# A chunked delta rule: full-array products with block masks against small row-tiled products, and inverses from two 16x16 blocks turned by VectorE

## The reference, cut to what matters

```
def _attn_ref(q, k, v, beta):          # 4 batches, 8 heads, 768 tokens, head dimension 48
    k_n = k / (np.linalg.norm(k, axis=-1, keepdims=True) + 1e-06)
    for t in range(S):
        y[:, :, t] = np.einsum('bhd,bhde->bhe', q[:, :, t], state)
        v_old = np.einsum('bhde,bhd->bhe', state, kt)
        state = state + bt[:, :, :, None] * np.einsum('bhd,bhe->bhde', kt, vt - v_old)
...
    x = attn_out as (3072 tokens, 384)
    x = _moe_ref(x, ...)               # x @ w_in, a rational function, @ w_out (384 -> 2048 -> 384)
    return _moe2_ref(x, ...)           # x @ w_in, h * tanh(softplus(h)), @ w_out
```

## Time and profile before

| what | value |
|---|---|
| runs shown | median 1323.81 us, 1314.73 to 1342.42, 3 runs |
| profiled execution | 1310.02 us, of which the span of the trace is 1308.0 us |
| start, to the first residual | 74 us |
| recurrence of 48 steps | 350.3 us |
| feed-forward | 883.7 us |
| busy in the span | TensorE 1151.2 us (88%), VectorE 933.4 (71%), ScalarE 739.5 (57%), GpSimd 194.9 (15%) |
| mean granted clock of TensorE | 0.925 |

### The profile page before, as it was taken

The page is one execution under the profiler, slowest core; times in us unless marked ns, Lnnn a source line. Parts: engine busy times, 40 slices in busy tenths (PEclk is TensorE's granted clock), DMA queues, the critical chain, the costliest instruction groups (busy, mean ns, idle before and its releaser), DMA issues.

```text
span 1308.0 us, 23511 instructions
## 1 busy us (share of the span) xinstructions
PE 1151.2 (88%) x9559; PEld 891.0 (68%) x9612; DVE 933.4 (71%) x1042; ACT 739.5 (57%) x932; POOL 194.9 (15%) x365
## 2 busy tenths in 40 slices
PE   5169697979899889998999999888999899989997
PEld 3146465657666667777777777667878787878875
DVE  2733343433444699998999999998878687768785
ACT  1124242413443777767777777776666566656664
POOL 1518646473820000000000000000000000000000
PEclk6569696958999999999999999999999899999999
DMA  6975565544462110001010102123010101010000
GB/s 141 208 154 121 128 133 143 126 112 111 105 199 64 37 49 18 31 1 48 0 48 0 49 1 82 40 73 97 1 49 1 49 0 48 1 48 1 23 2 25
DMA packets 81694, 83.82 MB, mean 64 GB/s; under 512 B 55040, under 2 KB 62720, under 8 KB 81024
## 3 DMA queue, kind: packets, MB, share of 16 engines
q1 hardware_dynamic: 70880, 60.43, 18.3%
q10 hardware_dynamic: 10720, 22.03, 6.1%
HBM read 61.99 MB, written 20.45 MB: 63 GB/s over the span
## 4 chain that ended last, share of the span: by engine, by line
DVE 31%; PE 29%; ACT 3%; issue 3%; DVEq 0%; ACTq 0%
PE o_ps L825 6%; PE o_ps L827 5%; PE o_ps L826 5%; DVE g_lo L1035 5%; DVE val L1029 5%; DVE val L997 4%; DVE val L1016 4%; PE h_ps L825 4%; PE h_ps L827 4%; PE h_ps L826 4%; DVE den L989 4%; DVE den L1024 4%; DVE pa L995 4%; ACT g_hi L895 1%; ACT stage L931 1%
## 5 line engine op out<-in xcount | busy, mean ns | idle before, releaser
L895 ACT ACTIVATE g_hi<-val 128x1024 fp32r<-128x1024 f32 x96 | 101.9, 1061 | 104.7 <-DVE val L1029 99.1
L825 PE MATMUL o_ps<-g_hi,w_hi_early 128*128 128x512 f32 x288 | 119.0, 413 | 32.2 <-DVE g_lo L1035 31.8
L825 PE MATMUL o_ps<-g_hi,w_hi_late 128*128 128x512 f32 x288 | 117.3, 407 | 22.5 <-DVE g_lo L1035 22.4
L681 DVE TENSOR_TENSOR u_blk<-hz_ps,w_blk 128x768 f32<-128x768 f32 x48 | 46.0, 958 | 116.7 <-PE hz_ps L390 116.7
L1029 DVE SCALAR_TENSOR_TENSOR val<-den,val 128x1024 f32<-128x1024 f32 x96 | 117.7, 1226 | 10.7 <-DVE den L1024 0.5
L525 ACT ACTIVATE stage<-y_ps 128x256 f32<-128x256 f32 x48 | 18.2, 379 | 183.9 <-PE y_ps L422 183.5
L1035 DVE SCALAR_TENSOR_TENSOR g_lo<-val,g_hi 128x1024 fp32r<-128x1024 f32 x96 | 117.6, 1225 | 5.8 <-ACT g_hi L895 5.7
L826 PE MATMUL o_ps<-g_lo,w_hi_early 128*128 128x512 f32 x288 | 116.1, 403 | 0.0
L827 PE MATMUL o_ps<-g_hi,w_lo_early 128*128 128x512 f32 x288 | 115.8, 402 | 0.0
L825 PE MATMUL h_ps<-x_hi,w_hi_early 128*128 128x512 f32 x288 | 112.4, 390 | 2.4 <-DVE val L997 2.0
L826 PE MATMUL o_ps<-g_lo,w_hi_late 128*128 128x512 f32 x288 | 114.3, 397 | 0.0
(11 more groups left out here) (96 smaller groups left out, 2368.5 us busy)
## 6 DMA issues: line engine op xcount, KB each, us to landing
w_raw<-w SPq DMA_DIRECT2D x14, 768.0 KB, 4.4
kq_gram<-kq_t SPq DMA_DIRECT2D x12, 768.0 KB, 11.4
x_raw<-x_dram SPq DMA_DIRECT2D x12, 768.0 KB, 5.5
kq_run<-kq_t ACTq DMA_DIRECT2D x40, 192.0 KB, 3.8
kv_run<-kv_n ACTq DMA_DIRECT2D x20, 384.0 KB, 5.3
k_norm<-kv_n SPq DMA_DIRECT2D x6, 768.0 KB, 4.7
x_dram<-stage ACTq DMA_DIRECT2D x24, 192.0 KB, 4.5
x_dram<-stage SPq DMA_DIRECT2D x6, 768.0 KB, 4.1
```

The source lines that it names most:

```text
L825: nc.tensor.matmul(dst, hi, rhs_hi, start=first, stop=False)
L895: act_fn(g_hi[:, n % 2], val[:, n % 2], ACT.Copy, scale=-1.0).then_inc(g_hi_ready, 1)
```

## The change

- The masks of blocks are gone (x_blk, u_blk, p_blk, w_blk, blk_mask and the work that made them). `solve`, `update` and `within` are instead written as 16 small products a step, one for each head and batch, whose operands lie at the 32 partitions of the batch (`quad(b)`). `update` and `within` are each cut into two halves of 8 products (batches 0 and 1, then 2 and 3), with the batches of a half in different PSUM banks.
- The 32x32 inverse is made from its two 16x16 diagonal blocks (`substitute`, 15 rounds, both blocks at once) and an off-diagonal block that TensorE makes in two products for each matrix (`side_join`, 64 products a call, four calls a tile) with a masked copy by ScalarE (`masked`) between and an addition by VectorE (`join`) behind.
- n_mat is turned into one matrix a partition, and the inverses back, by three VectorE transposes a tile (`turn_n`, `turn_z`, `turn_x`). n_dram and inv_dram are gone.
- The keys and queries are loaded once, in a ring of three tiles (kq), by SyncE, 4 chunks a tile. All loads and stores of the part are in SyncE's queue.
- No `keep_warm` is left in the recurrence. In the start there are 12 + 16 + 16.
- The loops over tiles are written out.
- y is stored to x1 in another order of batches, so a tile of x1 is loaded in pieces of 32 tokens (`load_x1`, 6 DMAs of 1024 pieces of 128 B), and a tile of x2 in 6 DMAs.

```diff
+    def load_x1(self, q, x1, t):
+        for k in range(KT):
+            tokens = self.x_raw[:, k].rearrange("p (m o t) -> p m o t", o=2, t=C)
+            stored = x1[P * k:P * k + P, t].rearrange("p (o m t) -> p m o t", o=2, t=C)
+            for o in range(2):
+                q.dma_start(tokens[:, :, o], stored[:, :, o]).then_inc(self.x_loaded, 16)
...
-            def hand_inverses(tau, first=False, following=True):
...
-                sp.wait_ge(inv_ready, tau + 3)
-                sp.dma_start(inv_dram, inv_x[:].rearrange("p i k -> p (i k)")).then_inc(inv_stored, 16)
...
-                        sp.dma_start(x_blk[C * b:C * b + C, c, :, C * b:C * b + C],
-                                     src[c, b]).then_inc(x_blk_loaded[c], 16)
...
+            for c in range(CT):
+                load_kq(0, c)
+            load_norm(1)
+            for c in range(CT):
+                load_kq(1, c)
+            for c in range(CT):
+                load_kv(0, c)
+            load_norm(2)
+            for c in range(CT):
+                load_kq(2, c)
+            for i in range(2):
+                w.load(sp, w1, i)
+            for tau in range(T):
+                if tau + 3 < T:
+                    load_norm(tau + 3)
...
                 for c in range(CT):
...
+                    if tau + 1 < T:
+                        sp.wait_ge(st_done, index(tau, c, 1) + 1)
+                        load_kv(tau + 1, c)
+                    if tau + RING < T:
+                        load_kq(tau + RING, c)
+                    if c == 1 and tau:
+                        store_y(tau - 1, 1)
+                    if c == 3:
+                        store_y(tau, 0)
+                if tau == 2:
+                    for cp in range(2):
+                        sp.wait_ge(hand.y_stored[cp], 64 + 64)
+                    hand.load_x1(sp, x1, 0)
...
+        def substitute(eng, tt, step, done):
...
+            for r in range(HC - 1, 0, -1):
+                shape = [P, 2, r, HC - r]
+                eng.wait_ge(step, done)
+                tt(inv_t[:, :, 0:r, r:HC], n[:, :, r, 0:r].unsqueeze(3).broadcast_to(shape),
+                   x[:, :, r, r:HC].unsqueeze(2).broadcast_to(shape), ALU.mult).then_inc(step, 1)
+                eng.wait_ge(step, done + 1)
+                tt(x[:, :, 0:r, r:HC], x[:, :, 0:r, r:HC], inv_t[:, :, 0:r, r:HC], ALU.subtract).then_inc(step, 1)
+                done += 2
...
+                pool.wait_ge(x_ready, j)
+                pool.wait_ge(eye_step, 5)
+                nc.gpsimd.tensor_copy(blocks(inv), eye[:]).then_inc(pool_step, 1)
+                pool.wait_ge(n_turned_ready, j + 1)
+                substitute(pool, nc.gpsimd.tensor_tensor, pool_step, STEPS * (j - 1) + 1)
...
+            def side_join(j, k):
...
+                for n in range(CG // 2):
+                    m = CG // 2 * h + n
+                    for b in range(B):
+                        left, right = ((n_mat[quad(b), j % 2, m], z_diag[quad(b), m]) if k % 2 == 0 else
+                                       (r_mat[quad(b), m], x_mat[quad(b), j % 2, m, HC:C]))
+                        last = nc.tensor.matmul(bg_ps[quad(b), 0, HC * n:HC * n + HC], left, right,
+                                                start=True, stop=True)
+                last.then_inc(bg_done, 1)
...
             def solve(tau, c, g):
...
-                for u in range(U):
-                    last = nc.tensor.matmul(hz_ps[:, u], x_blk[:, c, U * g + u], z[:, g, u],
...
+                for r in range(HALVES):
+                    for v in range(V):
+                        for b in range(B):
+                            last = nc.tensor.matmul(kh_ps[quad(b), r, P + D * v:P + D * v + D],
+                                                    x_mat[quad(b), tau % 2, HEADS * c + U * g + V * r + v],
+                                                    z[quad(b), V * r + v], start=True, stop=True)
                 last.then_inc(hz_done, 1)
...
             def q_state(tau, c, g):
...
+                for h in range(2):
+                    for v in range(V):
+                        for o in range(2):
+                            for r in range(HALVES):
+                                last = nc.tensor.matmul(y_at(r, v, 2 * h + o), state[rows(r), g, o, h, v],
+                                                        kq[rows(r), CT * (tau % RING) + c, 1, B * (V * g + v) + 2 * h + o],
+                                                        start=(h == 0 and v == 0), stop=False, skip_group_check=True)
...
+            def update(tau, c, g, h):
+                q = index(tau, c, g)
+                if h == 0:
+                    pe.wait_ge(u_ready, q + 1)
+                    pe.wait_ge(state_ready, q + 2)
+                else:
+                    pe.wait_ge(st_half, q + 1)
+                by_event()
+                for v in range(V):
                     for r in range(HALVES):
...
+                        for b in (2 * h, 2 * h + 1):
+                            at = V * D * h + D * v
+                            last = nc.tensor.matmul(st_ps[rows(r), b % 2, at:at + D], kv[quad(b), c, 0, U * g + V * r + v],
+                                                    u_row[quad(b), V * r + v], start=True, stop=True)
+                last.then_inc(st_done if h else st_half, 1)
+            def within(tau, c, g, h):
+                q = index(tau, c, g)
+                if h == 0:
+                    pe.wait_ge(q_done, q + 1)
...
+                    pe.wait_ge(y_half, q + 1)
+                by_event()
+                for v in range(V):
+                    for r in range(HALVES):
+                        for b in (2 * h, 2 * h + 1):
+                            last = nc.tensor.matmul(y_at(r, v, b), u_row[quad(b), V * r + v],
+                                                    p_mat[quad(b), tau % RING, HEADS * c + U * g + V * r + v],
+                                                    start=False, stop=True, skip_group_check=True)
+                last.then_inc(y_done if h else y_half, 1)
...
-                            gram_fill(tau + 2, G2 * c + g - FIRST_FILL)
-                        keep_warm(4)
-                        solve(tau, c, g)
-                        keep_warm(2)
-                        q_state(tau, c, g)
-                        keep_warm(1)
-                        update(tau, c, g)
-                        before = (c, g)
-                within(tau, *before)
...
+            keep_warm(12, bg_ps)
+            for c in range(CT):
+                early_gram(0, c)
+            pe.wait_ge(early_used, 1)
+            by_event()
+            keep_warm(16, bg_ps)
+            for c in range(3):
+                early_gram(1, c)
+            keep_warm(16, bg_ps)
+            for k in range(4):
+                side_join(0, k)
+                if k == 0:
+                    early_gram(1, 3)
...
+            pe.wait_ge(cleared, 4)
+            k_state(0, 0, 0)
+            for tau in range(T):
+                for s in range(NQ):
+                    c, g = s // G2, s % G2
+                    if s < CT and tau + 2 < T:
+                        side_gram(tau + 2, s)
+                    if s >= CT and tau + 1 < T:
+                        side_join(tau + 1, s - CT)
+                    solve(tau, c, g)
+                    q_state(tau, c, g)
+                    update(tau, c, g, 0)
+                    within(tau, c, g, 0)
+                    if s + 1 < NQ:
+                        k_state(tau, (s + 1) // G2, (s + 1) % G2)
+                    elif tau + 1 < T:
+                        k_state(tau + 1, 0, 0)
+                    within(tau, c, g, 1)
+                    update(tau, c, g, 1)
...
-            def spread_p(c, p):
-                for b in range(B):
-                    last = nc.scalar.activation(p_blk[:, c % 2, :, b], p[:, HEADS * c:HEADS * c + HEADS], ACT.Copy,
-                                                scale=blk_mask[:, b:b + 1])
...
+            def masked(j, h):
...
+                nc.scalar.activation(r_mat[:, CG // 2 * h:CG // 2 * h + CG // 2, 0:HC],
+                                     bg_ps[:, 0, 0:CG // 2 * HC].rearrange("p (n k) -> p n k", k=HC),
+                                     ACT.Copy, scale=lower_rows[:, 0:1]).then_inc(bg_used, 1)
...
+            def scale_gram(j, c, ps):
...
+                    dve_tt(part(n_mat[:, j % 2]), fill[:, 0], ws.unsqueeze(3).broadcast_to(shape), ALU.mult)
+                    last = dve_tt(part(p_mat[:, j % RING]), fill[:, 1],
+                                  upper[:].unsqueeze(1).unsqueeze(1).broadcast_to(shape), ALU.mult)
...
+            def turn_n(j):
...
+                nc.vector.transpose(square(n_turned), n_mat[:, j % 2].rearrange("p n k -> p k n")).then_inc(n_turned_ready, 1)
+            def turn_z(j):
...
+                nc.vector.transpose(z_diag[:].rearrange("p n i -> p i n"), square(inv)[:, 0:HC]).then_inc(z_diag_ready, 1)
+            def turn_x(j):
...
```

(70 more changed lines are left out.)

666 lines of the change are left out of this document (274 added, 392 removed).

## The result

The changed kernel takes 1317.22 us (median of 20 runs, 1311.31 to 1320.04), the kernel before beside it 1327.15 (median of 20, 1301.81 to 1349.25). The ratio of this kernel to the one before is 1.007 with a 95% interval of 1.004 to 1.010; it stands above 1, though the median is lower, because it leaves out runs in a slower state with a lower clock, which the kernel before fell into often. That is 0.7% slower and under the 2% that count as a change, where I had forecast 100 us less. The profiled execution took 1317.5 us, its span 1315.6.

What follows compares the result with a forecast made beforehand. TensorE was taken to bound the recurrence, forecast at 249 + 5 + 10 + 10 = 274 us instead of 350; with the start, 1310 - 76 - 26 = 1208 us, as a median 1222, range 1125 to 1290.

Steps and rivals of the forecast that it cites:

- The stops: Recurrence, TensorE waiting on "issue" in the written-out program of some 6,100 products: 10 us, bounds 0 and 53.
- the stops multiply: Rival, recurrence: stops of 4.4 us twice a tile, 53 us instead of 10, total 1265 us; chance 0.12.
- Products: Recurrence: TensorE's small products at half clock, gram products and off-diagonal groups included, take 249 us.
- products don't overlap in one bank: Rival, recurrence: products at different array rows writing one PSUM bank run one after another, 219 us more, 1441 us; chance 0.08.
- Clock: TensorE in the recurrence: stays at half clock, 1.2 GHz (0.50), giving 1222 us; chance 0.52.
- full-clock rival: Rival, recurrence: the dense stream keeps TensorE at 2.4 GHz, recurrence 185 us, total 1133 us; chance 0.22.
- VectorE and hand-overs: Recurrence: VectorE's work mostly hidden, 5 us showing; hand-overs and drains 0.2 us a step, 10 us.
- Not on the path: Rival, recurrence: another wait keeps the step as long as before, only the start's 26 us come, 1298 us; chance 0.06.
- Start: Before the recurrence: first residual at 48 us, 26 less than before, bounds 42 and 58.
- Feed-forward: Last stage: x1's loads in small pieces stay hidden and cost nothing; uncovered, up to 10 us in each of five tiles.
- The sum: Whole kernel: recurrence 76 us less and start 26 less give 1208 us profiled, 1222 us as a median.

Runs made afterwards that it cites:

- after: The changed kernel itself, against the kernel before it: median 1317.22 us, ratio 1.007.
- all_loop: Changed kernel's products reading fixed buffers, TensorE's recurrence looped over chunks of two steps, not the delta rule: 1204.99 us; the same written out 1309.77 us.
- wide7: Changed kernel with seven wide bf16 products of 512 columns added ahead of every step's side work: 1339.02 us, ratio 1.022.
- probe_stream: Changed kernel with five streams of small products, written out or looped, ahead of everything on TensorE; 1024 fp32 products took 78 us written out, 28.7 us looped.

## Why the prediction was wrong, point by point

- **The stops: the step that failed.** "The written-out program has some 6,100 products against a looped one ... I take 10 us, bounds 0 and 53." The changed recurrence lasts 369.6 us, the same products from a loop 260.2: the stops cost 109 us, twice the upper bound (107 us between the looped kernel and its own control). I had priced them as four rare events of the earlier trace rows and asked how often they would recur, in the rival *the stops multiply* as well (two a tile; "TensorE's program is read at some 130 products a step"). They are not events but a rate: 88 blocks of 256 instructions at 4.2 us each on average (3.5 to 4.0 in the probes), beside 1.9 us for running 64 small products. The rival came nearest to the mechanism, with half its size, since it kept the stop's 4.4 us and guessed the count. The count of blocks was in the diff (5632 x 4 / 256); the time that a block takes was in no row of before.
- **Products.** 249 us of them were forecast; the looped version holds them and every hand-over in 260. `solve` 0.81 (0.76), `q_state` 0.79 (0.89), `k_state` 0.50 (0.50), `update` 0.36 + 0.48 (1.04), gram 1.12 (1.0), off-diagonal groups 1.73 in the looped version (2.0): right within some tenths of a us, and *products don't overlap in one bank* (`solve` 3.0) falls. The Trainium skill (TensorEngine Tiling (Array Packing), "Restrictions and Gotchas", Gotcha 1) says that different row tiles can't access one PSUM bank at the same time. `solve` in 0.81 us disagrees with it, with four row places writing one bank; each of the four writes its own 32 partitions there, and products that share both bank and partitions weren't run.
- **Clock.** 0.50 as forecast, in after and in all_loop, where TensorE is busy 236.5 of 262.3 us. The full-clock rival didn't come, and wide7 with its 0.71 was no faster.
- **VectorE and hand-overs**, 5 + 10 us: 9.5 us of waits for VectorE in all_loop. The transposes were 1.9 to 2.0 us for 1024 elements and not 1.1, hidden as argued.
- **Not on the path.** This rival's 1298 us came nearest by number. That is luck: its mechanism, another wait of the chain between the engines, did not come. VectorE made TensorE wait 2.8 us.
- **Start.** First residual 59.21 us, forecast 48 (bounds 42 and 58). Part of it may be the same step: in the start's gram products TensorE stood 3.8 us at 18.6 and 6.3 us at 34.3 on "issue", while the loads ran (198 GB/s on average over the start). How much of that reached the first residual isn't shown, and the rest, three transposes at 0.9 us more each among it, I haven't split.
- **Feed-forward.** 885.1 us, with 883.7 forecast: the loads of x1 are hidden.
- **The sum.** 1208 for the profiled run, 1317.5 measured: +96 the recurrence, +11 the start, +3 the rest. As a median 1222 was forecast and 1317.2 measured.

Not tried: a looped recurrence that computes the reference. It would need each chunk's K and Q, keys, inverses and masked products brought to fixed buffers, and what those copies cost isn't known from these runs; 1205 us therefore shows what the supply costs, and isn't the time of a kernel that could be used.

## What to carry to other kernels

When a change turns few wide products into many small ones, count instructions before columns: a written-out stretch of TensorE took 3.5 to 4.2 us for each 256 instructions here, whatever they were (64 fp32 or 128 bf16 products). By these rows an fp32 product shorter than some 55 to 65 ns gained nothing by being shorter (an estimate, 3.5 and 4.2 us over 64). Stops of "issue" in the middle of a batch at equal numbers of records are the sign, and the packets of the instruction queue count the blocks. Either take products out, even at the price of more work on an idle engine (73 us here), or keep the program in a loop of at most some 1280 instructions (105 us here, in kernels whose loops read fixed buffers).

## What the runs showed of the hardware that wasn't expected

- A block took 3.46 to 4.01 us to come with the DMA queues quiet (probe_stream, fp32), and 7.85 to 8.95 us while the start's loads ran. The Trainium skill (Runtime: NRT & Kernel Launch, "Instruction fetch mechanics") says that programs are fetched in blocks of 256 instructions, ahead of execution, and that this stays hidden behind the rate of issue, and it holds full unrolling to be preferable. The size agrees with the 128 records and 128 loads between stops; that it stays hidden does not (1.90 us of work a block), and here unrolling cost 105 us.
- A loop kept its program up to 1280 instructions, with fp32 and with bf16 products; with fp32 it didn't at 1536. A body too long stands 4.5 to 4.8 us at its top (1536 instructions), a body that fits 0.2 us (the bf16 one of 1280).
- The clock stayed at 1.2 GHz (0.50) over 262 us in which TensorE was busy 90% with products of 16 to 64 columns (all_loop). It isn't so for every stream of small products: in probe_stream the four wide products took 1.89 us before the looped stream of 32 columns and 1.03 us behind it. What makes the difference isn't shown.
